# Token product by contraction halves, transposes two tiles behind, and the second attention step behind the third transposed tile

## What is computed

```python
for t in range(S):                       # attention, one state C (40 x 40) a head
    C = f_stab * C + i_stab * outer(v[t], k[t]);  n = f_stab * n + i_stab * k[t]
    y[t] = sigmoid(o_gate[t]) * (C @ q[t]) / max(abs(n @ q[t]), 1)
x = y as (768 tokens, 320)
h = relu(x.T @ w_tok1) @ w_tok2          # 768 -> 256 -> 768, mixes tokens
u = x + h.T
out = u + relu(u @ w_ch1) @ w_ch2        # 320 -> 1536 -> 320, mixes channels
```

## Time and profile before

| | us |
|---|---|
| median of 3 runs | 485.27 |
| profiled execution, time | 481.5 |
| its span | 479.8 |
| PE busy | 451.7 (94%) |
| DVE busy | 285.9 (60%) |
| ACT busy | 227.6 (47%) |
| POOL busy | 157.4 (33%) |
| batch 0, 1, 2, 3: first token product begins at | 62.98, 178.49, 286.15, 395.00 |

### The profile page before, as it was taken

One profiled execution on the slowest core, in us unless ns is written; L12 is line 12 of the kernel. 1 busy time (PEld: TensorE's weight loads), 2 busy tenths in 40 slices (PEclk: granted clock), 3 DMA queues, 4 the chain that ended last, 5 costly groups with the idle time before them and its releaser, 6 DMA issues.

```text
span 479.8 us, 9414 instructions
## 1 busy us (share of the span) xinstructions
PE 451.7 (94%) x3408; PEld 414.7 (86%) x3408; DVE 285.9 (60%) x660; ACT 227.6 (47%) x564; POOL 157.4 (33%) x212
## 2 busy tenths in 40 slices
PE   5988998788999999899999999899999999999996
PEld 3665787678999999789999999789999998899996
DVE  7476877777787425588787325587797324412312
ACT  2634557865655225865665125766555212212111
POOL 3424232546655001366655002266654000000000
PEclk9998799899999999999999999899999999999999
DMA  7499897224444302344454301344431001000101
GB/s 215 138 256 268 238 286 262 71 79 135 135 141 138 103 1 63 95 135 133 135 149 131 103 10 59 88 134 136 134 103 43 1 1 42 1 0 1 42 0 41
DMA packets 39189, 50.91 MB, mean 106 GB/s; under 512 B 3554, under 2 KB 31016, under 8 KB 39144
## 3 DMA queue, kind: packets, MB, share of 16 engines
q1 hardware_dynamic: 39144, 50.32, 35.2%
HBM read 46.27 MB, written 4.03 MB: 105 GB/s over the span
## 4 chain that ended last, share of the span: by engine, by line
PE 80%; ACT 6%; DVE 6%; issue 3%; DMA 3%; SPq 1%; POOL 0%; DVEq 0%; ACTq 0%; POOLq 0%
PE pC L952 30%; PE pA L1024 6%; PE pA L1025 6%; PE pA L1026 6%; PE pS L872 6%; PE pA L952 4%; PE pY L929 4%; PE pA L1028 3%; PE pA L1029 3%; DMA qd<-qT_dram 3%; PE pY L910 3%; PE pN L886 2%; PE pC L840 1%; DVE wc_lo L679 1%; PE pY L919 1%
## 5 line engine op out<-in xcount | busy, mean ns | idle before, releaser
L813 DVE SCALAR_TENSOR_TENSOR h_lo<-pA,h_hi 128x384 fp32r<-128x384 f32 x96 | 53.2, 554 | 119.0 <-ACT h_hi L615 119.0
L615 ACT ACTIVATE h_hi<-pA 128x384 fp32r<-128x384 f32 x96 | 46.7, 486 | 132.8 <-PE pA L1029 132.8
L952 PE MATMUL pC<-wc_hi,h_hi 128*128 128x320 f32 x288 | 94.0, 326 | 0.1
L952 PE MATMUL pC<-wc_lo,h_hi 128*128 128x320 f32 x288 | 89.0, 309 | 0.0
L952 PE MATMUL pC<-wc_hi,h_lo 128*128 128x320 f32 x288 | 88.6, 308 | 0.0
L422 POOL TENSOR_TENSOR gb<-gb,pb 128x384 f32<-128x384 f32 (+1 forms) x54 | 46.5, 862 | 112.1 <-ACT pb L529 111.9
L519 ACT ACTIVATE gb<-gb,aT 128x128 f32<-128x128 f32 x192 | 63.0, 389 | 14.3 <-POOL gb L433 14.3
L1024 PE MATMUL pA<-uT_hi,wc_hi 128*128 128x384 f32 x192 | 65.7, 342 | 2.5 <-DVE uT_hi L791 2.5
L1025 PE MATMUL pA<-uT_lo,wc_hi 128*128 128x384 f32 x192 | 65.0, 339 | 0.0
L1026 PE MATMUL pA<-uT_hi,wc_lo 128*128 128x384 f32 x192 | 64.7, 337 | 0.0
L952 PEld LDWEIGHTS pC<-wc_hi,h_hi 128*128 128x128 f32 x288 | 54.3, 189 | 0.9 <-issue 0.4
(11 more groups left out here) (113 smaller groups left out, 871.1 us busy)
## 6 DMA issues: line engine op xcount, KB each, us to landing
gb<-g_dram SPq DMA_DIRECT2D x23, 512.0 KB, 3.9
kv<-kvN_dram SPq DMA_DIRECT2D x24, 324.0 KB, 4.9
kd<-kT_dram SPq DMA_DIRECT2D x24, 180.0 KB
qz<-qT_dram SPq DMA_DIRECT2D x72, 60.0 KB
out_dram<-u SPq DMA_DIRECT2D x24, 160.0 KB, 1.9
gq<-g_dram SPq DMA_DIRECT2D x60, 60.0 KB
qd<-qT_dram SPq DMA_DIRECT2D x20, 180.0 KB, 5.1
x<-o_gate_dram SPq DMA_DIRECT2D x4, 640.0 KB, 4.5
```

The lines of the kernel that those rows point to most:

```text
L615: nc.scalar.activation(h2[0][:, slot % 2], pA[slot % 2][:, 0:HALF], ACT.Relu).then_inc(h2_hi, 1)
L813: nc.vector.scalar_tensor_tensor(h2[1][:, slot % 2], pA[slot % 2][:, 0:HALF], 0.0, h2[0][:, slot % 2].bitcast(F32), ALU.max, ALU.subtract) ...
L952: ins = mm(dst, a[p], b[q], start=first and n == 0, stop=last and n == 2)
```

## The change

The bank of a transposed tile, and on PE the second token product, its transposes and their waits:

```diff
-SECOND_AT = 3
...
+        def transposed_bank(s):
+
+            return pA[s % 2] if s < NC - 2 else pC[s - (NC - 2)]
...
-                    if s >= 2:
+                    if s < 2:
+                        pe.wait_ge(h1_lo, MT * b + s + 1)
+                    elif s < NC - 2:
                         pe.wait_ge(uT_lo, 2 * (NC * b + s - 1))
-                    else:
-                        pe.wait_ge(h1_lo, MT * b + s + 1)
...
-                for s in range(NC):
...
+                for m in range(MT):
+                    pe.wait_ge(h1_lo, MT * b + m + 1)
...
+                    for s in range(ST):
+                        ins = mixed(s, m)
+                        if m == MT - 1:
+                            ins.then_inc(t2_mm, 1)
+                transposes(0)
+                for s in range(ST, NC):
+                    pe.wait_ge(u_ready, NC * b + s - ST + 1)
                     for m in range(MT):
...
+                        ins = mixed(s, m)
                     ins.then_inc(t2_mm, 1)
-                    if s >= 1:
-                        transposes(s - 1)
-                    if more and s == SECOND_AT:
-                        attention(b + 1, 1)
-                transposes(NC - 1)
+                    if s < NC - 1:
+                        transposes(s - 2)
+                if more:
+                    attention(b + 1, 1)
+                transposes(NC - 3)
...
                     if slot < 2:
-                        pe.wait_ge(uT_lo, 2 * (NC * b + NC - 1 + slot))
+                        pe.wait_ge(uT_lo, 2 * (NC * b + ST + slot))
+                    if half == 1 and j == 0:
+                        pe.wait_ge(uT_lo, 2 * NC * (b + 1))
...
                     pe.wait_ge(h2_lo, k + 1)
+                    if j == 0 and half == 0:
+                        pe.wait_ge(uT_lo, 2 * NC * (b + 1))
...
                         hidden(slot)
+                    if slot == 0:
+                        transposes(NC - 2)
                     if more and slot < SLOTS:
                         attention(b + 1, slot + AHEAD)
+                    if slot == 0:
+                        transposes(NC - 1)
```

On ACT:

```diff
-                for s in range(NC + 1):
-                    if s < NC:
-                        act.wait_ge(u_ready, NC * b + s + 1)
-                        nc.scalar.activation(u[:, s, DM:3 * L], u[:, s, 2 * L:DM], ACT.Copy).then_inc(u_twice, 1)
-                    if s == 0:
-                        continue
-                    s -= 1
+                def u_high(s):
                     act.wait_ge(uT_mm, NC * b + s + 1)
-                    src = pA[s % 2][:, 0:3 * L].rearrange("p (t s) -> p t s", t=3)
+                    src = transposed_bank(s)[:, 0:3 * L].rearrange("p (t s) -> p t s", t=3)
                     nc.scalar.activation(uh[:, :, s * L:(s + 1) * L], src, ACT.Copy).then_inc(uT_hi, 1)
-                    if more and s + 1 == SECOND_AT:
-                        attention(b + 1, 1)
+
+                for s in range(NC):
+                    act.wait_ge(u_ready, NC * b + s + 1)
+                    nc.scalar.activation(u[:, s, DM:3 * L], u[:, s, 2 * L:DM], ACT.Copy).then_inc(u_twice, 1)
+                    if s >= ST:
+                        u_high(s - ST)
+                if more:
+                    attention(b + 1, 1)
+                u_high(NC - 3)
...
-                    if more and slot == 0:
-                        sigmoid(b + 1)
+                    if slot == 0:
+                        u_high(NC - 2)
                     if more:
                         attention(b + 1, slot + AHEAD)
+                    if slot == 0:
+                        u_high(NC - 1)
+                        if more:
+                            sigmoid(b + 1)
```

On DVE:

```diff
-                    if s >= 2:
-                        u_low(s - 2)
-                    if more and s == SECOND_AT:
-                        attention(b + 1, 1)
+                    if s >= ST:
+                        u_low(s - ST)
+                if more:
+                    attention(b + 1, 1)
+                u_low(NC - 3)
                 if more:
                     p_low(b + 1, 0)
-                for s in range(NC - 2, NC):
-                    u_low(s)
...
+                    if slot == 0:
+                        u_low(NC - 2)
                     if b == 0:
                         for n in slot_pieces(slot):
                             split_lo(n)
                     if more and slot < SLOTS:
                         attention(b + 1, slot + AHEAD)
+                    if slot == 0:
+                        u_low(NC - 1)
```

More of the change, by code:

```diff
@@ L788, in u_low @@
                     cols = slice(s * L, (s + 1) * L)
[L789 removed]
+                    bank_s = transposed_bank(s)
+                    nc.vector.tensor_tensor(ul[:, :, cols], bank_s[:, 0:2 * L].rearrange("p (t s) -> p t s", t=2),
                                             uh[:, 0:2, cols].bitcast(F32), ALU.subtract).then_inc(uT_lo, 1)
[L791 removed]
+                    nc.vector.tensor_tensor(uh[64:128, 2, cols], bank_s[64:128, 2 * L:3 * L],
                                             uh[64:128, 2, cols].bitcast(F32), ALU.subtract).then_inc(uT_lo, 1)
@@ L984, in transposes @@
                     pe.wait_ge(u_twice, NC * b + s + 1)
-                    nc.tensor.transpose(pA[s % 2][:, 2 * L:3 * L], u[:, s, 2 * L:3 * L], ident[:, :]).then_inc(uT_mm, 1)
+                    nc.tensor.transpose(bank_s[:, 2 * L:3 * L], u[:, s, 2 * L:3 * L], ident[:, :]).then_inc(uT_mm, 1)
                 if more:
                     attention(b + 1, 0)
-                for s in range(NC):
-                    if s < ST:
-                        if b != 0:
-                            pe.wait_ge(out_ready, 2 * ST * b)
-                    else:
-                        pe.wait_ge(u_ready, NC * b + s - ST + 1)
-                    for m in range(MT):
-                        if s == 0:
-                            pe.wait_ge(h1_lo, MT * b + m + 1)
-                            if b == 0:
-                                pe.wait_ge(w_lo, 2 + m + 1)
-                        ins = split_products(pC[s % ST][:, 0:DM], [w[:, m, s * L:(s + 1) * L] for w in wt2],
-                                             [a[:, m] for a in h1], m == 0, m == MT - 1)
-                    ins.then_inc(t2_mm, 1)
-                    if s >= 1:
-                        transposes(s - 1)
-                    if more and s == SECOND_AT:
-                        attention(b + 1, 1)
@@ L1008, in batch, with mixed @@
-                transposes(NC - 1)
+                def mixed(s, m):
+                    return split_products(pC[s % ST][:, 0:DM], [w[:, m, s * L:(s + 1) * L] for w in wt2],
+                                          [a[:, m] for a in h1], m == 0, m == MT - 1)
+                if b != 0:
+                    pe.wait_ge(out_ready, 2 * ST * b)
+                for m in range(MT):
+                    pe.wait_ge(h1_lo, MT * b + m + 1)
+                    if b == 0:
+                        pe.wait_ge(w_lo, 2 + m + 1)
+                    for s in range(ST):
+                        ins = mixed(s, m)
+                        if m == MT - 1:
+                            ins.then_inc(t2_mm, 1)
```

5 lines of the change are left out of this document (2 added, 3 removed).

## The result

The changed kernel takes 498.5 us (median of 4 runs, 496.95 to 502.96); the kernel before 483.37 (4 runs, 478.15 to 486.87). The ratio is 1.035, 95% interval 1.030 to 1.041: slower. The profiled execution took 497.87, its span is 496.1.

A forecast was written before the change was run, and what follows sets the result against it. PE was taken as the bound (80% of the chain, busy 94%). Batch losses 5.3 + 3.9 + 3.9 + 1.4 = 14.5 us on 481.5 gave 496.0, plus 3 for low clock 499; range 490 to 505.

The forecast's parts named there:

- Step 1: Second token product by contraction halves: wins the 0.61 us wait for h1_lo in batch 3, but sums come late.
- Step 2: Transposes two tiles behind: those of tile 2 wait for u_low(0), as ACT's high part follows a copy; new gap 1.1 us.
- Step 3: First hidden product, batch 1: starts at 194.30 after u_low(2), PE waiting 1.45 us, yet 0.74 earlier than before.
- Step 4: From hidden(0) to hidden(1), batch 1: values(0) waits for p_low(0) as attention step 1 comes late; gap 0.9 us.
- Step 5: Start of project(0), batch 1: ACT waits for POOL's rest(1), scores 3 and tile 5 come late; 2.0 us later.
- Step 6: Slots 1 and 2, batch 1: later table load makes ACT 3.9 us late; gaps 0.9 at scores 4, 1.7 at values(2).
- Batch 0: Late tiles queue around the weight splits on ACT and DVE: scores 3 go 3.5 us later, the batch grows by 5.3.
- The clock: PE's granted clock falls after wider handoff gaps: two more low stretches of 1.7 us each, counted as +3 us.
- Nothing takes the gaps' place: Handoff waits vanish and the rest stays: 1.45 us won a batch, 475.7 us; chance 0.04.
- Half absorbed: ACT catches up in the slots and only project(0)'s delay counts: 7.4 us, 489; chance 0.07.
- No change: What hidden(0) gains pays for the rest, ACT's high part of slot 0 keeping its time: 481 to 484; chance 0.04.
- Clock in every handoff: PE's clock falls in each batch's widened handoff: 496.0 + 4 x 1.7 and more, 503 or more; chance 0.08.

The follow-up runs named there:

- the edit on ACT alone: Changed kernel with ACT's high part of tile s - 3 put ahead of the copy of tile s; median 487.56 us, 1.013 of the kernel before.
- the banks alone: Kernel before with only tiles 4 and 5 transposed into pC0 and pC1, no engine's list changed; median 476.8 us, ratio 0.988.
- the tiles are ahead: Changed kernel with tiles 4 and 5 handed over ahead of hidden(0) on PE, ACT and DVE; ratio 1.018 to the kernel before.

## Why the prediction was right, point by point

The direction and the time hold, and so do most steps. The forecast was worked out for the profiled execution: 499.0, where 497.9 was measured, and the median is 498.5. As a difference, 17.5 was forecast over the profiled execution of before, and 16.4 came.

- *Step 1, halves.* It held: the 0.61 of batch 3 went, and alone the step can't be measured in the times.
- *Step 2, transposes of tile 2.* The high part of tile 0 was forecast 5.40 us after the scores of step 0 (189.01 less 183.61) and came at 5.40; the transposes were forecast at 6.80 (190.41 less 183.61) and came at 6.80 (196.26 less 189.46). The cause was shown by the edit on ACT alone. The gap reads 0.92 and not 1.1 since the profile counts it from the end of the matmul before, and the prediction from the end of its turn, 0.15 us earlier.
- *Step 3, `hidden(0)`.* 10.69 was forecast, 10.66 measured.
- *Step 4, `values(0)`.* 14.02 was forecast, 14.39 measured. Everything up to the start of `p_low(0)` was on time (13.40 forecast, 13.36 measured). Then `p_low(0)` took 0.75 and not 0.56, beside POOL's mask (202.16 to 203.84), which this step leaves out. And PE started 0.28 behind its end, not the 0.06 that the prediction takes; why, no run shows. The 0.4 was absorbed: scores 3 wait for DVE and not for `values(0)`, and go at 17.24 where 17.19 was forecast.
- *Step 5, `project(0)`.* 18.79 was forecast, 18.85 measured. POOL's `rest(1)` made ACT wait as said (0.24).
- *Step 6, sigmoid.* The high part of slot 1 was forecast at 20.9 to 21.0 and measured at 20.95, `values(2)` at 25.4 and at 25.46. The sentence that the gap is "behind the sigmoid" invites a wrong remedy: in the changed kernel, the sigmoid put back wins nothing.
- *The wakes.* The reason given for the wake of 0.15 us, that the waited tile is PE's stationary operand, does not hold. The transposes of tile 2 start 0.15 behind the low part, for which they wait only to have the bank free; in the kernel with the banks alone the transposes that wait for `u` itself start 0.06 behind it. The number was right where the forecast used it.
- *Batch 0.* Scores 3 were forecast at 88.2 and came at 88.60, measured from the same start. 0.2 of the 0.4 was there from the transposes of tile 2 on (7.02 after the scores of step 0, where the working for batch 1 has 6.80). The high part of slot 1 came 5.7 later than before where 5.3 was forecast, and the batch grew by 5.7.
- *Batch 3.* Gaps of 0.9, 0.6, 1.4 and 0.6 stand in the places forecast, each 0.2 under its forecast as in step 2; `project(0)` is at 14.37 where 14.3 was forecast, and the batch grew by 1.7 for 1.4.
- *The clock.* This is the term that was mis-sized. Two more low stretches were put in at +3. The changed kernel's trace has two more: four (two in batch 0, one each in 1 and 2) for the two of before, 6.8 us of work lost for 3.4. But the sum without the clock was 14.5 and the batches grew by 16.2, so 1.7 is left for the clock: a low stretch costs less time than work where part of it lies in waits. Nor did every widened gap bring one: in batches 1 and 2 the clock is 1.00 over the gaps of 0.92, 1.27 and 1.08, and falls only at the gap of 1.80 at `values(2)`. So the number of stretches has luck in it, and so has a point within 0.5 of the median: the four runs of before alone range over 8.7 us.
- *The rivals.* Nothing takes the gaps' place: no. The high part of tile 0 came at 189 and not before 188, which that rival needed; with that one order mended, it came 4.2 after the scores of step 0 (187.8), and both gaps did vanish. Half absorbed: no, the loss of `project(0)`, 2.1 in batch 1, had grown to 4.1 at `project(1)`. No change: no, ACT's high part of slot 0 came 1.75 later. Clock in every handoff: no, no batch has its low stretch between the transposes of tile 2 and `hidden(0)`; three of the four batches have one further on.

What stays open: what the sigmoid's place alone costs once the tiles are ahead, which a trace tells (1.1 us of ACT's time a batch) and no edit; why `values(0)` starts 0.28 behind `p_low(0)`; and why the same gap brings the low clock in one batch and not in another.

## What to carry to other kernels

Deferring a hand-over on one engine reorders every in-order list that it passes through: before moving it, write out for each engine what the instruction now stands behind, for here one copy in front of a read, with its wait for a later tile, cost 7 us, and two lines in the other order gave them back. A change can hold a good part and two bad ones: the banks alone, with no list moved, gained about 1% where the whole lost 3.5%. And where an engine has a block of work in the way, shrinking the block (tanh in the table that exp has loaded, in place of sigmoid) gained what moving it did not.
